# Attention and two MLP layers on one core: the order of the loads in the first chunk, and the lower parts of seven weight groups

## The reference

```python
keep = is_sink | in_window            # 4 sink keys, window 128; q, k, v: (2, 8, 768, 64)
scores = np.where(keep, scale * q @ k.T, -1e9)
a = exp(scores - max); a = a / (sum(a) + 1e-9)
x = (a @ v) as (1536, 512)            # 2 x 768 tokens, 8 heads x 64

h = x @ w_in                          # w_in (512, 2048), w_out (2048, 512)
x = where(h >= 1, h, where(h <= -1, 0, (h + 1)**2 / 4)) @ w_out
h = x @ w_in2
y = where(h > 0, h, exp(min(h, 0)) - 1) @ w_out2
```

## Time and profile before

| | |
|---|---|
| median of three runs | 657.24 us |
| profiled execution: time | 661.64 us |
| profiled execution: span in the profile | 659.9 us |
| busy in the span: PE, DVE, ACT, POOL | 637.5, 378.4, 349.8, 9.3 us |
| granted clock of TensorE over the span | 0.99 of full |
| first chunk, first ramp (L668) to the first ramp of the second chunk | 28.72 to 101.24 us |
| second chunk, likewise | 101.24 to 161.58 us |

### The profile page before, as it was taken

How to read it: one execution, slowest core, us unless ns; L and a number is a source line. 1 busy time by engine, 2 the same in 40 slices (tenths; PEclk the granted TensorE clock), 3 DMA queues, 4 the chain that set the end, 5 groups by cost and what they waited for, 6 DMA issues and landing times.

```text
span 659.9 us, 12209 instructions
## 1 busy us (share of the span) xinstructions
PE 637.5 (97%) x4164; PEld 565.3 (86%) x4164; DVE 378.4 (57%) x994; ACT 349.8 (53%) x830; POOL 9.3 (1%) x27
## 2 busy tenths in 40 slices
PE   5787999999999999999999999999999999999998
PEld 3686989999999999999999988888888888888886
DVE  6697877886887788678857864322332222322221
ACT  5686756765666576557655663333443333533333
POOL 3000000000000000000000000000000000000000
PEclk9798899999999999999999999999999999999999
DMA  8564212330232133123144510000010000100001
GB/s 284 157 230 150 66 41 63 88 102 25 63 100 62 29 96 86 38 62 86 38 159 133 182 39 0 1 0 1 24 40 0 0 0 0 64 0 0 0 0 64
DMA packets 24314, 42.47 MB, mean 64 GB/s; under 512 B 2752, under 2 KB 13536, under 8 KB 24288
## 3 DMA queue, kind: packets, MB, share of 16 engines
q1 hardware_dynamic: 24288, 42.13, 20.4%
HBM read 38.98 MB, written 3.15 MB: 64 GB/s over the span
## 4 chain that ended last, share of the span: by engine, by line
PE 89%; DVE 7%; ACT 2%; issue 1%; DMA 1%; SPq 0%; ACTq 0%; DVEq 0%
PE h_ps L505 13%; PE h_ps L507 13%; PE h_ps L506 13%; PE y_ps L520 10%; PE y_ps L522 9%; PE y_ps L521 9%; PE s_ps L520 3%; PE s_ps L522 3%; PE s_ps L521 3%; PE o_ps L488 3%; PE t_ps L468 2%; PE s_ps L458 1%; PE s_ps L459 1%; DVE wout_lo L838 1%; PE o_ps L490 1%
## 5 line engine op out<-in xcount | busy, mean ns | idle before, releaser
L505 PE MATMUL h_ps<-x_hi,win_hi 128*128 128x256 f32 (+1 forms) x576 | 188.8, 328 | 0.4
L507 PE MATMUL h_ps<-x_hi,win_lo 128*128 128x256 f32 (+1 forms) x576 | 184.8, 321 | 0.0
L506 PE MATMUL h_ps<-x_lo,win_hi 128*128 128x256 f32 (+1 forms) x576 | 184.4, 320 | 0.0
L520 PE MATMUL y_ps<-g_hi,wout_hi 128*128 128x256 f32 (+1 forms) x480 | 148.2, 309 | 1.4 <-DVE g_lo L851 1.4
L522 PE MATMUL y_ps<-g_hi,wout_lo 128*128 128x256 f32 (+1 forms) x480 | 146.3, 305 | 0.0
L521 PE MATMUL y_ps<-g_lo,wout_hi 128*128 128x256 f32 (+1 forms) x480 | 146.1, 304 | 0.0
L868 DVE SCALAR_TENSOR_TENSOR g_full<-g_full,h_ps 128x512 f32<-128x512 f32 x48 | 32.9, 686 | 156.7 <-ACT g_full L673 156.7
L505 PEld LDWEIGHTS h_ps<-x_hi,win_hi 128*128 128x128 f32 x576 | 109.3, 190 | 10.3 <-DVE g_full L864 1.0
L507 PEld LDWEIGHTS h_ps<-x_hi,win_lo 128*128 128x128 f32 x576 | 109.5, 190 | 9.5
L506 PEld LDWEIGHTS h_ps<-x_lo,win_hi 128*128 128x128 f32 x576 | 109.8, 191 | 8.5
L660 ACT CAST g_hi<-g_full 128x256 fp32r<-128x256 f32 (+1 forms) x144 | 68.5, 476 | 68.5 <-DVE g_full L868 34.1
(11 more groups left out here) (105 smaller groups left out, 739.4 us busy)
## 6 DMA issues: line engine op xcount, KB each, us to landing
ks<-in_k SPq DMA_DIRECT2D x40, 260.0 KB, 2.7
raw<-in_w_in SPq DMA_DIRECT2D x11, 512.0 KB, 4.7
raw<-in_w_out SPq DMA_DIRECT2D x11, 512.0 KB, 4.4
qs<-in_q SPq DMA_DIRECT2D x40, 128.0 KB, 2.6
vals<-in_v SPq DMA_DIRECT2D x20, 192.0 KB
out_y<-xy SPq DMA_DIRECT2D x12, 256.0 KB, 2.1
xy<-in_w_in SPq DMA_DIRECT2D x5, 512.0 KB, 5.9
xy<-in_w_out SPq DMA_DIRECT2D x5, 512.0 KB, 4.7
```

What stands on the lines that cost most here:

```text
L505: pe.matmul(o, win_hi[:, k, f], x_hi[:, k, :], start=(k == 0), stop=False)
L506: pe.matmul(o, win_hi[:, k, f], x_lo[:, k, :], start=False, stop=False)
L507: last = pe.matmul(o, win_lo[:, k, f], x_hi[:, k, :], start=False, stop=(k == KT - 1))
L520: pe.matmul(o, wout_hi[:, t, cols], g_hi[:, t % GR, :], start=begin, stop=False, skip_group_check=True)
```

## The change

Two things are changed. First, `BY_POOL` = groups 3, 5, 7, 9, 11, 13 and 15 (the `w_out` groups 1 to 7 of the first layer): DVE's `split_weights` returns at once for them, and GpSimd does the same subtraction instead, as two instructions of 128x512 for each group, as soon as ACT has made the upper part. They count on a semaphore of their own, `pool_w_lo_ready`, and TensorE and SP wait for it where the group is such a one (`splits_done`). GpSimd does them after the mask copy of L407 and before that of L412. Second, SP's order is written anew: heads 4, 5, 6, 7 and the values move up between the weight groups, `load_weights(5)` stands ahead of the values of pair 0, `load_weights(7)` ahead of head 2, and groups 9 to 11 ahead of head 3.

```diff
+BY_POOL = list(range(EARLY, NW, 2))
+
+        def splits_done(i):
+            if i in BY_POOL:
+                return pool_w_lo_ready, (BY_POOL.index(i) + 1) * 2
+            return w_lo_ready, i + 1 - len([b for b in BY_POOL if b < i])
...
                 if splits_until_free(i) > 0:
-                    sp.wait_ge(w_lo_ready, splits_until_free(i))
+                    sp.wait_ge(*splits_done(splits_until_free(i) - 1))
...
             load_head(1, 0)
             load_head(1, 1)
+            load_weights(5)
             load_values(1, 0)
-            load_weights(5)
+            load_values(1, 1)
             load_weights(6)
+            load_weights(7)
             load_head(1, 2)
-            load_weights(7)
+
             load_weights(8)
+            load_weights(9)
+            load_weights(10)
+            load_weights(11)
             load_head(1, 3)
-            load_values(1, 1)
-            load_weights(9)
-            for i in range(10, NW):
-                load_weights(i)
-            load_pair(1, 2)
-            load_pair(1, 3)
+            load_weights(12)
+            load_weights(13)
+            load_head(1, 4)
+            load_weights(14)
+            load_head(1, 5)
+            load_weights(15)
+            load_values(1, 2)
+            load_head(1, 6)
+            load_head(1, 7)
+            load_values(1, 3)
...
+            for i in BY_POOL:
+                hi, lo = w_parts(order[i])
+                src = split_source(i)
+                pool.wait_ge(w_hi_ready, i + 1)
+                for k in range(2):
+                    nc.gpsimd.tensor_tensor(lo[:, k, :], src[:, k, :], hi[:, k, :].bitcast(F32), ALU.subtract).then_inc(pool_w_lo_ready, 1)
...
             def split_weights(i):
-                n = order[i]
+                if i in BY_POOL:
+                    return
                 dve.wait_ge(w_hi_ready, i + 1)
```

More of the change, by code:

```diff
@@ L168, in build @@
         g_ready, g_lo_ready, x_lo_ready, w_lo_ready = sem("g_ready"), sem("g_lo_ready"), sem("x_lo_ready"), sem("w_lo_ready")
+        pool_w_lo_ready = sem("pool_w_lo_ready")
         mask_step, mask_ready = sem("mask_step"), sem("mask_ready")
@@ L256, in build, with split_source @@
         at = {n: i for i, n in enumerate(order)}
+        def splits_done(i):
+            if i in BY_POOL:
+                return pool_w_lo_ready, (BY_POOL.index(i) + 1) * 2
+            return w_lo_ready, i + 1 - len([b for b in BY_POOL if b < i])
+        def split_source(i):
+            return raw_buffer(i).rearrange("p (k f) -> p k f", k=KT if order[i] % 2 == 0 else 2)
         def splits_first(t):
@@ L495, in hidden @@
                 pe.wait_ge(w_hi_ready, at[layer * NW + 2 * (t // 2)] + 1)
-                pe.wait_ge(w_lo_ready, at[layer * NW + 2 * (t // 2)] + 1)
+                pe.wait_ge(*splits_done(at[layer * NW + 2 * (t // 2)]))
                 if t >= 2:
@@ L510, in outward @@
             def outward(layer, c, t):
-                pe.wait_ge(w_lo_ready, at[layer * NW + 2 * (t // 2) + 1] + 1)
+                pe.wait_ge(*splits_done(at[layer * NW + 2 * (t // 2) + 1]))
                 pe.wait_ge(g_lo_ready, c * FT + (t + 1))
@@ L640, in split_weights @@
                         act.wait_ge(y_step, (NC - 1) * FT + 2 * (m // 2) + 2)
-                src = raw_buffer(i).rearrange("p (k f) -> p k f", k=KT if n % 2 == 0 else 2)
-                nc.scalar.copy(w_parts(n % NW)[0], src).then_inc(w_hi_ready, 1)
+                nc.scalar.copy(w_parts(n % NW)[0], split_source(i)).then_inc(w_hi_ready, 1)
             def split_x(layer, c, at_chunk):
@@ L833, in split_weights @@
             def split_weights(i):
-                n = order[i]
+                if i in BY_POOL:
+                    return
                 dve.wait_ge(w_hi_ready, i + 1)
-                hi, lo = w_parts(n % NW)
-                src = raw_buffer(i).rearrange("p (k f) -> p k f", k=KT if n % 2 == 0 else 2)
-                nc.vector.tensor_tensor(lo, src, hi.bitcast(F32), ALU.subtract).then_inc(w_lo_ready, 1)
+                hi, lo = w_parts(order[i] % NW)
+                nc.vector.tensor_tensor(lo, split_source(i), hi.bitcast(F32), ALU.subtract).then_inc(w_lo_ready, 1)
             def split_x(layer, c, at_chunk):
```

## The result

The changed kernel is slower, by a third of a percent. Over 20 runs each it took 660.75 us (median) and the kernel before 658.77 us; the ratio of the runs is 1.0036, 95% interval 1.0022 to 1.0050 (that of the two medians is 1.0030). The forecast was 656.5 us, 0.7 us less than before. The size lies within the half percent that I called the same, but outside the forecast's own range of 654 to 659 us; the sign is wrong, and the interval leaves no room for a gain.

The account below looks back on a forecast made before the run. TensorE bounds later chunks; DVE and head 4's late load hold up the first, with 12.2 us to win. Loads -4.2, removal -5.7, block +9.2 gave -0.7 us: 656.5 us from 657.24, own range 654 to 659, 8-in-10 range 647 to 663.

Parts of the forecast that it names:

- the loads: First chunk: head 4 issued near 47 us instead of 56.50 ends DVE's wait and the low clock; gain 4.2 us.
- the stop: First chunk: TensorE's longest wait for DVE's split of a head, 3.6 us, traced back to the late load of head 4.
- The removal: First chunk: seven splits of 1.14 us leave DVE, five of them counted on its path; gain 5.7 us.
- the other two: Splits in the first chunk, groups 9 and 15, hidden by waits for ACT's exponentials; removal worth about nothing.
- the five: Splits of groups 3, 5, 7, 11 and 13 in the first chunk, all on DVE's path; removal worth 5.7 us.
- steps 6 and 12: First-chunk steps where a normalisation behind the split waits for ACT's exponentials anyway; removing these splits worth about nothing.
- The block: First chunk: GpSimd's SBUF reads shut out DVE's two-SBUF-input instructions; 0.66 us per half, fourteen cost 9.2 us.
- Rival 1: First chunk: GpSimd works beside DVE at no cost, so 9.9 us come off; 647.3 us, chance 0.13.
- Rival 2: First chunk: halves are short or fall into DVE's own waits, costing 5.2 us; 652.5 us, chance 0.22.
- Rival 3: First chunk: each second half cuts in ahead of DVE, fourteen cost 15.8 us; slower, 663.1 us, chance 0.19.
- Rival 4: First chunk: SP stands at buffers awaiting GpSimd, so head 4 isn't earlier; 660.7 us, chance 0.06.

Follow-up runs that it names:

- lower_zeroed: Changed kernel with GpSimd filling the seven lower parts with zeros instead of subtracting; 652.70 us, first chunk (C, first ramp to first ramp) 64.52 us.
- before_again: The kernel before, unchanged, run and profiled again; 657.19 us, first ramp (F) at 25.43 us, first chunk (C) 71.21 us.
- loads_only: Changed kernel with the new order of loads but all splits on DVE; 654.12 us, ratio 0.9930 to before, first chunk (C) 68.25 us.
- after_third: The changed kernel, unchanged, profiled a third time; 660.63 us (one run), first ramp (F) at 25.61 us, first chunk (C) 74.59 us.
- whole_groups: Changed kernel with one GpSimd subtraction of 128x1024 per group instead of two of 128x512; 662.13 us, ratio 1.0055 to before.

## Why the prediction was wrong

**What bounds the kernel, and the loads.** Right in kind: the stop and the low clock behind it are gone, head 4 goes out at 47.9 us. I counted 4.2 us. Against the execution that I had read, the loads alone gave 4.3 us. Against one with a full opening they gave 3.0 us, since the low clock behind the stop was milder there. The term held for the profile and was 1.2 us too large for executions with a full opening. Its agreement with the profile is in part luck: of the 1.2 us that I counted for the low clock, 0.63 us was a wait of DVE that its row puts to ACT's cast of a group (L642) and not to TensorE.

**The removal.** This is the step that failed most. I put 5 x 1.14 = 5.7 us on DVE's path and nothing on the other two. The two were worth 0.35 us, near enough; the five were worth 3.3 us. The error is in "come off DVE's path": I looked for what hides a split only in steps 6 and 12, by the instruction behind it, and didn't ask in the other five how soon ACT's next product was due. ACT makes the upper part of the same group, then that of the next head, just ahead of DVE. With the five gone DVE waited 1.8 us more for ACT (1.3 us for a head's upper parts, 0.5 us for `g_hi`), which is most of the 2.4 us that were missing; the rest is open.

**The block.** Right, and the best of the sum: 9.2 us forecast, 9.3 us of growth in the changed kernel, 9.0 us on the chunk when measured alone. Between lower_zeroed and the changed kernel with a full opening lie 10.1 us of C, of which the new fall of the clock at 34 to 42 us is a part. A half took about 1.2 us, against 1.13 (the shortest pair 2.52 us, a whole group in one instruction 2.37 us). The 1.13 itself was loosely made: twice the copy's 0.63 us less 0.1 is 1.16, and no row shows the fixed cost of 0.1 us. Its own length stayed hidden as argued.

**The sum.** By the measured terms, with a full opening, it is -3.0 - 3.7 + 10.1 = +3.4 us. The terms are steps from one C to the next, from before_again over loads_only and lower_zeroed to after_third, so that they add up to the whole distance in C is no proof of them. The forecast was -0.7. Of the 4.1 us between the two 2.0 are the removal, 1.2 the loads and 0.9 the block, some 0.5 of that the new fall of the clock. The lower end of the forecast's own range was also off by 1 us: -5.7 - 5.7 + 9.2 = -2.2 us leads to 655.0 us and not to 654.

**From the profile to the median.** Profile against profile the forecast looked nearly right: both spans are 659.9 us, +0.0 against -0.7. That is luck, since both openings had fallen. I noted that the profiled execution lay 4.4 us above the median of the runs, and carried the difference over as if it were the same for both kernels. It was not. It was made of a slow opening and a longer low clock behind the stop; the change takes away the second and, in the profiles, most of what the first costs. The medians over all openings differ by 2.0 us, between the 0 of fallen and the 3.6 of full ones. Why the opening falls in some executions and not in others is open, and so is whether the change alters how often.

**The rivals.** Rival 1 (no block) falls by the growth of DVE's forms. Even lower_zeroed, where hardly anything blocks and which leaves seven lower parts out, took 650.6 us at its shortest, 3 us more than the 647.3 us of this rival. Rival 2 (short halves, 5.2 us in all) falls by the same 9.3 us. Rival 3 had the right sign and mechanism and too high a price: each half cost 0.65 to 0.72 us, not 0.94 or more. I had put the break-even at 0.71 us a half. With the measured gains of 3.0 + 3.7 = 6.7 us it is 6.7 / 14 = 0.48 us, and that is what turned the sign. Rival 4 (SP stuck at GpSimd's buffers) falls by head 4's issue at 47.9 us.

## What to carry to other kernels

Work handed to an idle GpSimd isn't free for DVE where it reads SBUF: price each instruction as one block of its own length, times the share of DVE's work that has two SBUF inputs, and compare it with what the removal is worth. Price a removal by the next wait in each place, not by the length of what is removed. Where a profile lies some microseconds off the median, find out in which stage before carrying the difference over to the changed kernel.

## What the runs showed of the hardware

An instruction on two elements of each partition can carry a block of 1.1 us: the small `TENSOR_SCALAR` of the maxima at 64.83 us in the changed kernel took 1.10 us instead of 0.17. And a fill on GpSimd, which reads nothing, left DVE's subtractions at 420 and 694 ns but stretched this `TENSOR_SCALAR` from a mean of 169 to 337 ns.

The granted clock of TensorE in the same opening, of the same kernel, stayed at 1.00 in one execution and fell to 0.50 in another, and F was 3.3 us longer there. Of this 1.0 us came earlier, where the clock reads 1.00 in both and the same eight matmuls took 1.65 us in the one and 0.98 in the other. The three profiles that fell only at 20 us (before, after, whole_groups) all have 1.65 us for these eight; those with a full opening have 0.93 to 1.46. Of the 49 runs of the kernel before that stood beside the first eight experiments, 29 lay above 658.5 us and 20 below.
